# Taking a turn's outputs before the range steps of the next cosine argument

## The chip, the cores and the metric

One NeuronCore of a Trainium2 chip runs the whole program in one launch. The metric is device time in microseconds. The time before is 681.76 us, the median of 3 runs (681.07, 681.76 and 683.96).

## The reference, cut to what matters

Three stages follow each other on 1152 tokens (2 batches of 576) of width 512:

```
scores = q @ k.T / 8, kept for 0 <= i - j < 64      # sliding window attention, 8 heads of 64
x = softmax(scores) @ v                              # (1152, 512)

p = domain_probs / (sum(domain_probs) + 1e-9)        # 4 experts
x = sum over e of  p[:, e] * (relu(x @ w1[e]) @ w2[e])    # w1 512x1024, w2 1024x512

h = x @ w_in                                         # 512 -> 2048
out = (h * cos(h)) @ w_out                           # 2048 -> 512
```

## The kernel before, in words

Every product is done in three passes of a split format: each operand is a high part (fp32r) and a low part (the rest), and hi*hi + hi*lo + lo*hi are summed in PSUM. ScalarE makes the high parts by a copy (`w_hi` L418, `hp_hi` L423), VectorE or GpSimd the low parts by a subtraction (`hp_lo` L550 on VectorE, `w_lo` L314 on GpSimd).

After the attention the work goes in 18 turns of 3 token tiles (384 tokens each) by 6 blocks of weights: blocks 0 to 3 are the experts, blocks 4 and 5 are the two halves of the last layer (the cosine blocks). A turn is called (block, tile). It has 8 chunks of 128 hidden rows, and each chunk has an "up" product of 12 matmuls of 384 columns (L721) into one of four PSUM banks, and a "down" product (12 matmuls L749 in an expert turn, 9 matmuls of 512 columns L752 in a cosine turn) that adds to the turn's outputs in the other four banks. TensorE runs three chunks ahead: in its iteration f (0 to 7) of a turn it does the up product of chunk f+3, which for f of 5 and more belongs to the next turn, and then the down product of chunk f. I call the chunk whose up product is done in iteration f "the chunk of iteration f"; its down product comes three iterations later.

Within a cosine chunk the work passes between engines. ScalarE scales and rounds the argument (`c_u`, L428). VectorE does the three range steps: it takes the rounding constant off (`c_k`, L583), and subtracts the multiple of two pi in two parts (`c_r1` L585, `c_r2` L588). ScalarE takes the absolute value (L435) and the sine (L437), VectorE multiplies by h (`h_raw`, L596). The split of this chunk into `hp_hi` (ScalarE, L423) and `hp_lo` (VectorE, L550) is issued one iteration late: ScalarE does it behind the `c_u` of the following chunk, VectorE behind the following chunk's `c_r2`. All these orders are written out by hand, and each engine's queue is in order.

At the end of a turn VectorE moves the outputs from PSUM to the accumulator `acc` (`take_outputs`): a copy (L575) in the first block of a layer, an addition (L577) in the others, 4 pieces of 384 columns in an expert turn and 3 of 512 in a cosine turn. They wait for the turn's last down product (`down_done`). The first down product of the next turn waits for `y_taken` of the bank it writes, and for `hp_lo` of its chunk. In a turn followed by cosine work in its iteration 7 (these are (3,2), (4,0), (4,1), (4,2), (5,0) and (5,1)) `take_outputs` is called from inside `times_cosine`, between the previous chunk's `hidden_low` and the wait for the sine.

In the last tile of a block the next block's weights are refilled: ScalarE does `high_weights(f - 1)` in iteration f behind `hidden_high`, and ahead of the absolute value and sine; the eighth one, `high_weights(FC - 1)` (L456), comes behind the sine of iteration 7 and ahead of the next turn's first `c_u`. GpSimd makes each `w_lo` when its `w_hi` is there. Behind the eight `w_lo` of block 4, GpSimd also makes the input of the last layer for tile 2: `next_input(2)`, a cast to `x_hi` (L363) and a subtraction to `x_lo` (L365), both over 1536 columns. In front of block 4's eight it has done the same for tiles 0 and 1.

All tiles of the cosine steps (`c_u` to `c_cos`) and `acc` are parts of one SBUF tensor, so the profile calls them `arena`.

Of the kernel before, what the change touches and what calls it, by code (L numbers as in the profile page):

```python
# [34 lines left out]
FC = F1 // P  # L35
# [45 lines left out]
def build(nc, q, k, v, probs, weights, out):  # L81
    with ExitStack() as ctx:
# [418 lines left out]
        def _(dve):  # L501
# [46 lines left out]
            def hidden_low(f, s):  # L548
                dve.wait_ge(hp_hi_done, s + 1 + C_HI)
                nc.vector.tensor_tensor(hp_lo[:, f % HP, :], h_raw[:, f % HP, :], hp_hi[:, f % HP, :],  # L550
                                        ALU.subtract).then_inc(hp_lo_done, 1)
# [12 lines left out]
            def take_outputs(e, turn, t, mix, last=False):  # L564
                if isinstance(e, int) and e == E:
                    dve.wait_ge(x2_lo_done, t + 1)
                if not last:
                    dve.wait_ge(down_done, turn * FC + FC + C_DOWN)
                for c in range(DC if mix else OC):
                    if last:  # L570
                        dve.wait_ge(result_done, c + 1)
                    n = TOK if mix else DM
                    cell = acc[:, ds1(t), c * n:(c + 1) * n]
                    if isinstance(e, int) and e in (0, E):
                        nc.vector.tensor_copy(cell, y_ps[c][:, 0:n].unsqueeze(1)).then_inc(y_taken, 1)  # L575
                    else:
                        nc.vector.tensor_tensor(cell, y_ps[c][:, 0:n].unsqueeze(1), cell, ALU.add).then_inc(y_taken, 1)  # L577

            def times_cosine(f, s, late, take=None):
                n = s - MIX * FC  # L580
                bank_h = h_ps[f % HB][:, 0:TOK]
                dve.wait_ge(cos_u, n + 1)
                nc.vector.tensor_scalar_sub(c_k, c_u, ROUND).then_inc(cos_k, 1)  # L583
                dve.wait_ge(cos_k, n + 1)
                nc.vector.scalar_tensor_tensor(out=c_r1, in0=c_k, scalar=-TWO_PI_HI, in1=bank_h,  # L585
                                               op0=ALU.mult, op1=ALU.add).then_inc(cos_r1, 1)
                dve.wait_ge(cos_r1, n + 1)
                nc.vector.scalar_tensor_tensor(out=c_r2, in0=c_k, scalar=-TWO_PI_LO, in1=c_r1,  # L588
                                               op0=ALU.mult, op1=ALU.add).then_inc(cos_r, 1)
                if late:  # L590
                    hidden_low((f - 1) % FC, s - 1)
                if take is not None:
                    take_outputs(*take)
                dve.wait_ge(cos_done, n + 1)
                dve.wait_ge(hp_hi_done, s - HP + 1 + C_HI)
                nc.vector.tensor_tensor(h_raw[:, f % HP, :], c_cos, bank_h, ALU.mult).then_inc(h_taken, 1)  # L596

            def dve_turn(e, t, turn, mix_now, mix_next, last=False):
                for f in range(FC):
                    g, s = (f + LAG) % FC, turn * FC + f + LAG  # L600
                    own = f < FC - LAG
                    if last and not own:
                        if f == FC - LAG:
                            hidden_low(FC - 1, s - 1)
                    elif mix_now if own else mix_next:
                        wrap = isinstance(t, int) and t == NTOK - 1
                        share(g, s, e if own or not wrap else e + 1, t if own else 0 if wrap else t + 1)
                    else:
                        times_cosine(g, s, not (isinstance(s, int) and s == MIX * FC),
                                     (e, turn, t, mix_now) if f == FC - 1 else None)  # L610
                if mix_next or last:
                    take_outputs(e, turn, t, mix_now, last)
# [16 lines left out]
            for f in range(FC):  # L629
# [17 lines left out]
                if f != FIRST:  # L647
                    s = f + FIRST if f < FIRST else f + LAG
# [194 lines left out]
def ds1(i):  # L843
    return bass.ds(i, 1)
# [37 lines left out]
```

## Time and profile before

| what | value |
|---|---|
| median of 3 runs | 681.76 us (681.07 to 683.96) |
| the profiled execution's own time | 683.99 us |
| its span | 682.2 us |
| TensorE matmul busy | 649.3 us (95%), 3960 instructions |
| VectorE busy | 319.0 us (47%), 718 instructions |
| ScalarE busy | 237.7 us (35%), 511 instructions |
| GpSimd busy | 156.2 us (23%), 100 instructions |
| mean granted TensorE clock | 0.982 of full speed |
| chain that ended last, by engine | PE 90%, DVE 3%, ACT 3%, POOL 3%, issue 2% |

PE is TensorE, PEld its weight loads, DVE VectorE, ACT ScalarE, POOL GpSimd. Times in rows are in us from the start of the span unless marked ns. The span is 1.8 us shorter than the execution's own time. The cosine turns begin near 480 us; the last one ends with the span.

### The profile page before, as it was taken

What the parts mean: (1) busy time and instruction counts of PE and PEld (TensorE: products, weight loads), DVE (VectorE), ACT (ScalarE), POOL (GpSimd) and SP (SyncE); (2) the same over time, 40 slices, a digit from 0 to 9 for tenths busy, and PEclk for the clock granted to TensorE, in tenths of its full rate; (3) what the DMA queues carried; (4) which work ended last, traced back from release to release, by engine and by line L of the source; (5) the groups of instructions that cost most, each with busy time, mean ns of one, the idle gap of its engine ahead of it and who ended that gap; (6) DMA issues with size and microseconds to landing.
All of it is one profiled execution on the core that took longest, in us unless ns stands there. A gap on an engine that the chain in (4) does not pass through costs nothing.

```text
span 682.2 us, 10822 instructions
## 1 busy us (share of the span) xinstructions
PE 649.3 (95%) x3960; PEld 617.4 (91%) x3960; DVE 319.0 (47%) x718; ACT 237.7 (35%) x511; POOL 156.2 (23%) x100
## 2 busy tenths in 40 slices
PE   5867789999999999999999999999999999899998
PEld 4757679999999999999999999999899999799996
DVE  4542264232423232423232423234866688866664
ACT  5752352113211113311123211126455466544453
POOL 6632210005500015400015303055600025300000
PEclk9987899999999999999999999999999999899999
DMA  9961130003400003300004200003200003001011
GB/s 286 302 222 49 62 135 1 1 1 104 144 0 1 0 0 124 123 0 0 0 10 138 99 1 0 0 32 123 93 2 0 1 32 92 1 1 47 0 46 47
DMA packets 21684, 39.59 MB, mean 58 GB/s; under 512 B 2064, under 2 KB 13328, under 8 KB 21648
## 3 DMA queue, kind: packets, MB, share of 16 engines
q1 hardware_dynamic: 21564, 39.08, 17.6%
q8 instruction: 23, 0.38, 0.2%
q14 instruction: 13, 0.11, 0.1%
q10 hardware_dynamic: 84, 0.02, 0.0%
HBM read 36.72 MB, written 2.38 MB: 57 GB/s over the span
## 4 chain that ended last, share of the span: by engine, by line
PE 90%; DVE 3%; ACT 3%; POOL 3%; issue 2%; POOLq 0%; ACTq 0%; DVEq 0%
PE bank L721 43%; PE bank L749 29%; PE bank L752 14%; POOL w_lo L314 2%; PE bank L713 2%; PE bank L700 1%; ACT w_hi L418 1%; ACT arena L394 1%; DVE hp_lo L550 0%; PE bank L685 0%; POOL mask L291 0%; DVE arena L583 0%; DVE arena L588 0%; DVE arena L525 0%; DVE arena L577 0%
## 5 line engine op out<-in xcount | busy, mean ns | idle before, releaser
L721 PE MATMUL bank<-x_hi,w_hi 128*128 128x384 f32 (+1 forms) x576 | 197.7, 343 | 11.6 <-POOL w_lo L314 11.3
L721 PE MATMUL bank<-x_hi,w_lo 128*128 128x384 f32 (+1 forms) x576 | 195.3, 339 | 0.0
L721 PE MATMUL bank<-x_lo,w_hi 128*128 128x384 f32 (+1 forms) x576 | 195.1, 339 | 0.0
L314 POOL TENSOR_TENSOR w_lo<-w_raw,w_hi 128x1024 fp32r<-128x1024 f32 (+1 forms) x52 | 117.4, 2261 | 331.0 <-ACT w_hi L418 325.3
L423 ACT ACTIVATE hp_hi<-h_raw 128x384 fp32r<-128x384 f32 x144 | 75.0, 523 | 304.3 <-DVE h_raw L556 282.8
L556 DVE SCALAR_TENSOR_TENSOR h_raw<-bank,p_bc 128x384 f32<-128x384 f32 x96 | 53.3, 557 | 179.7 <-PE bank L721 178.7
L749 PE MATMUL bank<-hp_hi,w_hi 128*128 128x384 f32 x384 | 130.8, 341 | 1.8 <-DVE hp_lo L550 1.8
L749 PE MATMUL bank<-hp_lo,w_hi 128*128 128x384 f32 x384 | 128.9, 336 | 0.0
L749 PE MATMUL bank<-hp_hi,w_lo 128*128 128x384 f32 x384 | 128.8, 335 | 0.0
L721 PEld LDWEIGHTS bank<-x_hi,w_hi 128*128 128x128 f32 x576 | 109.9, 191 | 15.8 <-POOL w_lo L314 12.3
L550 DVE TENSOR_TENSOR hp_lo<-h_raw,hp_hi 128x384 fp32r<-128x384 f32 x144 | 91.1, 635 | 69.6 <-ACT hp_hi L423 69.6
L721 PEld LDWEIGHTS bank<-x_lo,w_hi 128*128 128x128 f32 x576 | 110.0, 191 | 1.9
L721 PEld LDWEIGHTS bank<-x_hi,w_lo 128*128 128x128 f32 x576 | 109.8, 191 | 0.0
L749 PEld LDWEIGHTS bank<-hp_hi,w_hi 128*128 128x128 f32 x384 | 72.7, 189 | 2.6 <-DVE hp_lo L550 2.0
L749 PEld LDWEIGHTS bank<-hp_lo,w_hi 128*128 128x128 f32 x384 | 72.7, 189 | 0.0
L749 PEld LDWEIGHTS bank<-hp_hi,w_lo 128*128 128x128 f32 x384 | 72.5, 189 | 0.0
L752 PE MATMUL bank<-w_hi,hp_hi 128*128 128x512 f32 x144 | 56.9, 395 | 4.4 <-DVE arena L575 2.8
L752 PE MATMUL bank<-w_lo,hp_hi 128*128 128x512 f32 x144 | 57.4, 399 | 0.0
L752 PE MATMUL bank<-w_hi,hp_lo 128*128 128x512 f32 x144 | 57.4, 398 | 0.0
L418 ACT ACTIVATE w_hi<-w_raw 128x1024 fp32r<-128x1024 f32 x44 | 46.1, 1047 | 0.1
L435 ACT ACTIVATE arena<-arena 128x384 f32<-128x384 f32 x48 | 25.2, 525 | 55.6 <-DVE arena L588 55.6
L596 DVE TENSOR_TENSOR h_raw<-arena,bank 128x384 f32<-128x384 f32 x48 | 26.5, 552 | 33.7 <-ACT arena L437 33.7
(46 smaller groups left out, 468.4 us busy)
## 6 DMA issues: line engine op xcount, KB each, us to landing
w_raw<-in_weights SPq DMA_DIRECT2D x44, 512.0 KB, 3.5
arena<-in_q SPq DMA_DIRECT2D x12, 192.0 KB, 4.8
p_bc<-p_scratch SPq DMA_DIRECT2D x4, 576.0 KB, 6.7
result<-arena SPq DMA_DIRECT2D x9, 256.0 KB, 2.1
w_raw<-in_weights SPq DMA_DIRECT2D x8, 256.0 KB, 5.6
arena<-in_k SPq DMA_DIRECT2D x8, 224.0 KB, 4.6
arena<-in_v SPq DMA_DIRECT2D x4, 384.0 KB, 3.6
arena<-in_v SPq DMA_DIRECT2D x4, 320.0 KB, 6.6
```

Of the source, the lines that this page charges most:

```text
L314: return nc.gpsimd.tensor_tensor(w_lo[:, f, cols], w_raw[:, f % STAGE, cols], w_hi[:, f, cols], ALU.subtract)
L394: last = nc.scalar.activation(prob[:, g % PR, t, :], s_sb[:, g % 2, t, :], ACT.Exp, bias=neg_max[:, g % PR, t:t + 1], scale=-1.0, accum_ou ...
L418: nc.scalar.activation(w_hi[:, f, :], w_raw[:, f % STAGE, :], ACT.Copy).then_inc(w_hi_done, 1)
L423: nc.scalar.activation(hp_hi[:, f % HP, :], h_raw[:, f % HP, :], ACT.Copy).then_inc(hp_hi_done, 1)
L435: nc.scalar.activation(c_abs, c_r2, ACT.Abs).then_inc(cos_abs, 1)
L550: nc.vector.tensor_tensor(hp_lo[:, f % HP, :], h_raw[:, f % HP, :], hp_hi[:, f % HP, :], ALU.subtract).then_inc(hp_lo_done, 1)
L556: nc.vector.scalar_tensor_tensor(out=h_raw[:, f % HP, :].unsqueeze(1), in0=ps[:, 0:TOK].unsqueeze(1), scalar=0.0, in1=p_bc[:, ds1(e), toke ...
L596: nc.vector.tensor_tensor(h_raw[:, f % HP, :], c_cos, bank_h, ALU.mult).then_inc(h_taken, 1)
L713: last = nc.tensor.matmul(o_bank(m)[heads, block_of * WIN:(block_of + 1) * WIN], v_w[:, r, WINDOW_OF[t][block_of], heads], prob_t[:, h, bl ...
L721: last = nc.tensor.matmul(ps[:, 0:TOK], w[:, f, chunk(c)], x[:, c, token_cols(t)], start=c == 0 and i == 0, stop=c == DC - 1 and i == 2)
L749: product = nc.tensor.matmul(y_ps[c][:, 0:TOK], w[:, f, DM + c * P:DM + (c + 1) * P], h[:, f % HP, :], **flags)
L752: product = nc.tensor.matmul(y_ps[c][:, :], h[:, f % HP, chunk(c)], w[:, f, DM:2 * DM], **flags)
```

## The change

`times_cosine` is called with `take` in iteration 7 of the six turns named above. There, the low part of the previous chunk and then the outputs are now done ahead of the three range steps; before, they came behind them. Nothing is added or removed, and no other engine's order is written differently.

```diff
             def times_cosine(f, s, late, take=None):
                 n = s - MIX * FC
                 bank_h = h_ps[f % HB][:, 0:TOK]
+                if take is not None:
+                    hidden_low((f - 1) % FC, s - 1)
+                    take_outputs(*take)
                 dve.wait_ge(cos_u, n + 1)
                 nc.vector.tensor_scalar_sub(c_k, c_u, ROUND).then_inc(cos_k, 1)
...
                 nc.vector.scalar_tensor_tensor(out=c_r2, in0=c_k, scalar=-TWO_PI_LO, in1=c_r1,
                                                op0=ALU.mult, op1=ALU.add).then_inc(cos_r, 1)
-                if late:
+                if late and take is None:
                     hidden_low((f - 1) % FC, s - 1)
-                if take is not None:
-                    take_outputs(*take)
                 dve.wait_ge(cos_done, n + 1)
```

## Rows read from the trace of the kernel before

**Rows 1.** Waits of PE from 440 us on: total us, times, longest us.
```profile
PE bank L752 <- DVE arena L575: 2.8, 1, 2.8
PE bank L752 <- DVE arena L577: 1.6, 1, 1.6
```
**Rows 2.** Timeline of PE, end of turn (3,2): start us, us, instruction, idle before.
```profile
479.82 0.34 PE L721 MATMUL bank<-x_hi,w_lo 128*128 128x384 f32 x1
481.71 0.47 PE L752 MATMUL bank<-w_hi,hp_hi 128*128 128x512 f32 x1 [1.55 <-DVE arena L577]
...
490.16 0.39 PE L752 MATMUL bank<-w_hi,hp_hi 128*128 128x512 f32 x1
```
**Rows 3.** Timeline of DVE, end of turn (3,2) and the two chunks after.
```profile
477.87 0.56 DVE L588 SCALAR_TENSOR_TENSOR arena<-arena 128x384 f32<-128x384 f32 x1
478.35 2.75 DVE L550 TENSOR_TENSOR hp_lo<-h_raw,hp_hi 128x384 fp32r<-128x384 f32 x1
481.02 1.94 DVE L577 TENSOR_TENSOR arena<-bank,arena 128x384 f32<-128x384 f32 x4
...
485.60 3.19 DVE L588 SCALAR_TENSOR_TENSOR arena<-arena 128x384 f32<-128x384 f32 x1
488.71 0.55 DVE L550 TENSOR_TENSOR hp_lo<-h_raw,hp_hi 128x384 fp32r<-128x384 f32 x1
```
**Rows 4.** Timeline of ACT, end of turn (3,2).
```profile
476.42 0.52 ACT L423 ACTIVATE hp_hi<-h_raw 128x384 fp32r<-128x384 f32 x1
...
479.02 0.62 ACT L437 ACTIVATE arena<-arena,half_pi 128x384 f32<-128x384 f32 x1
479.55 1.04 ACT L418 ACTIVATE w_hi<-w_raw 128x1024 fp32r<-128x1024 f32 x1
480.49 0.47 ACT L428 ACTIVATE arena<-bank 128x384 f32<-128x384 f32 x1
```
**Rows 5.** Timeline of POOL, end of turn (3,2).
```profile
477.96 5.39 POOL L314 TENSOR_TENSOR w_lo<-w_raw,w_hi 128x1024 fp32r<-128x1024 f32 x2 [0.93 <-ACT w_hi L418]
483.30 1.47 POOL L363 CAST x_hi<-arena 128x1536 fp32r<-128x1536 f32 x1
484.85 3.52 POOL L365 TENSOR_TENSOR x_lo<-arena,x_hi 128x1536 fp32r<-128x1536 f32 x1
```
**Rows 6.** Timeline of DVE, end of turn (4,1).
```profile
547.24 1.88 DVE L575 COPY arena<-bank 128x512 f32 x3
549.03 0.54 DVE L596 TENSOR_TENSOR h_raw<-arena,bank 128x384 f32<-128x384 f32 x1
```
**Rows 7.** Timeline of POOL in the refill of turn (4,2), two of its eight.
```profile
555.09 2.39 POOL L314 TENSOR_TENSOR w_lo<-w_raw,w_hi 128x1024 fp32r<-128x1024 f32 x1 [66.72 <-ACT w_hi L418]
...
571.93 2.39 POOL L314 TENSOR_TENSOR w_lo<-w_raw,w_hi 128x1024 fp32r<-128x1024 f32 x1 [0.65 <-ACT w_hi L418]
```
**Rows 8.** Timeline of DVE in the refill of turn (4,2) and at its end.
```profile
569.79 0.56 DVE L596 TENSOR_TENSOR h_raw<-arena,bank 128x384 f32<-128x384 f32 x1 [0.78 <-ACT arena L437]
...
572.13 2.60 DVE L588 SCALAR_TENSOR_TENSOR arena<-arena 128x384 f32<-128x384 f32 x1
...
575.98 0.55 DVE L596 TENSOR_TENSOR h_raw<-arena,bank 128x384 f32<-128x384 f32 x1 [0.77 <-ACT arena L437]
...
579.23 0.55 DVE L596 TENSOR_TENSOR h_raw<-arena,bank 128x384 f32<-128x384 f32 x1 [0.78 <-ACT arena L437]
...
584.54 1.87 DVE L575 COPY arena<-bank 128x512 f32<-128x512 f32 x3
```
**Rows 9.** Timeline of PE, end of turn (4,2).
```profile
582.09 0.34 PE L721 MATMUL bank<-x_hi,w_lo 128*128 x1
585.27 0.80 PE L752 MATMUL bank<-w_hi,hp_hi 128*128 128x512 f32 x1 [2.84 <-DVE arena L575]
...
588.98 0.34 PE L721 MATMUL bank<-x_hi,w_hi 128*128 x1
```
**Rows 10.** Windows: stretch, length, busy us of each engine, granted clock, DMA.
```profile
585.20:588.40 3.20, 3.13 (x7) 2.49 (x8) 3.20 (x5) 1.99 (x4) 2.03 (x1) 0.50 0.02 5
```

## The prediction

> **What bounds the kernel now.** I read the busy shares first (matmuls 95% of the span, the chain of waits 90% on PE), then PE's own waits behind 440 us, since only the six boundaries named in the change are touched, and then the timelines of PE, DVE, ACT and POOL at each of them. A DVE edit moves the time only where PE waits for DVE. Behind 440 us PE does so twice [rows 1]: 1.6 us at the end of turn (3,2), and 2.8 us at the end of turn (4,2). The reader should see in both that the first down product of the next turn waits for its bank to be taken. At the other four boundaries PE does not wait.
>
> Why DVE is late there is seen beside POOL. An `hp_lo` costs 0.55 us, but the one at 478.35 took 2.75: a POOL `w_lo` had begun at 477.96 [rows 3, 5]. A `c_r2` costs 0.56, but took 3.19 at 485.60, ending 0.42 behind the end (488.37) of the `x_lo` begun at 484.85 [rows 3, 5]. So a DVE step with both inputs in SBUF waits for the running POOL operation and ends 0.42 after it; `c_k` (one input, 0.36 long) is held too and, as in the profile's other cases, I take it to end 0.22 after. The `c_r2` at 477.87 had started when `w_lo` came, and the `hp_lo` asked for at 478.35, while that `c_r2` ran, was still served behind `w_lo`: an operation of POOL that arrives during a DVE step goes ahead of the DVE step behind it. The takes, which read PSUM, are not held: four in 1.94 us while `w_lo` ran.
>
> **Boundary (3,2) to (4,0), what is gained.** The last up product before the wait starts its last matmul at 479.82, and the next product would follow 0.17 behind, at 479.99; it came at 481.71 [rows 2]. With the change `hp_lo` needs only `hp_hi`, which is ready at 476.94 [rows 4], and ends near 477.5, ahead of `w_lo`. The takes start when the last down product is finished, about 478.2. The first takes about 0.55, so the bank is free by 478.8, ahead of 479.99. The whole 1.72 us goes: two up-down pairs took 490.16 - 481.71 = 8.45 [rows 2], so the third down product of the turn, that of the chunk of iteration 7, could start at 479.99 + 8.4 = 488.4.
>
> **The same boundary, what is late next.** The takes end at 480.1, and only then do the range steps come. `c_k` is asked for at 480.1 while `w_lo` runs from 477.96 to 480.35, and ends at 480.57. `c_r1` and `c_r2` (0.59 each from start to start) end at 481.75; absolute value and sine at 482.95. Behind this sine stands the last `w_hi` of the block: sine at 479.02 and `w_hi` at 479.55 before [rows 4], sine at 482.33 and `w_hi` at 482.86 after, so 3.3 us late. That is the price, for three things queue behind it. POOL's last `w_lo`, then its cast and `x_lo`, run one after another from there: `w_lo` 483.98 to 486.37, cast to 487.95, `x_lo` to about 491.75 (2.39, 1.5 and 3.7 with the gaps, of [rows 5] with a little for DVE steps between them). ACT's next `c_u` comes 0.94 behind `w_hi` [rows 4], at 483.8, and is ready at 484.27, too late to get `c_k` in before `w_lo`. So `c_k` ends at 486.59, `c_r1` at 487.18; `c_r2` is asked for during the cast and ends at 488.37; `x_lo` arrives during it, at 488.03, and goes ahead of the `hp_lo` behind it. This `hp_lo`, of the chunk of iteration 7, ends at 491.75 + 0.42 = 492.2. Before, it ended at 489.26 [rows 3], ahead of its use at 490.16. Now PE wants it at 488.4 and waits 3.8 us. That product starts at 492.2 instead of 490.16: +2.05 us, the 1.72 gained being already in it.
>
> The wait also touches the clock. In front of 585.27 PE had stood for 2.84 us, and behind it the granted clock was 0.50, that is 1.2 GHz, for 3.2 us [rows 9, 10]: nine matmuls took 588.98 - 585.27 = 3.71 instead of 2.08, so 1.63 us lost. In front of 481.71 it had stood for 1.55 and lost nothing of that kind (two pairs in 8.45). A wait of 3.8 is nearer to the first: I add 1.6; the ends are 0 and 3.3 (twice it).
>
> A rule of the Trainium skill bears on the held steps: SBUF — State Buffer, section Who interferes with whom, says that VectorE and GpSimd share a pair of ports, that whoever issues first has it for its whole instruction, and that the other blocks fully. The order in [rows 3, 5] agrees. By the rule taken at its word a held `hp_lo` would add its full 0.55 behind POOL and not 0.42; the sum of this boundary would then be about 0.4 higher for its three held steps.
>
> **The four boundaries without POOL work,** (4,0), (4,1), (5,0), (5,1): the takes start 0.25 earlier, which nobody waits for, and `h_raw` of that chunk comes 2.5 us later. At (4,1): takes at 547.0, `c_k` 1.79 later (547.24 to 549.03 [rows 6]) at 548.8, `h_raw` at 551.55 instead of 549.03. Its down product is three iterations of 4.19 later, with over 3 us to spare, and a late chain gains 0.9 us a chunk. Cost 0; were that cover gone, 2.5 each.
>
> **Boundary (4,2) to (5,0).** Here PE stands from 582.26 (0.17 behind 582.09) to 585.27, and with the clock this costs 4.6 us [rows 9]. Taken alone, the edit removes it: `hp_lo` and the first take would be done by 581.9. But the refill in turn (4,2) starts from a chain 2.5 us late, and I followed it chunk by chunk. A late chunk is of two kinds. Clear: `h_raw` to next `h_raw` 3.25 (575.98 to 579.23). Blocked: 6.19 (569.79 to 575.98), because `w_lo` begins 2.14 behind the first `h_raw` (571.93) and `c_r2` is asked for at 2.34 (572.13) [rows 7, 8]. The kinds alternate: the `w_lo` begun in a clear chunk holds the next one's `c_k` for a microsecond, which puts its `c_r2` behind the next `w_lo`. Before, the first `w_lo` came at 555.09 [rows 7] and iterations 3 and 5 were blocked; iteration 6 was clear, with `h_raw` at 579.23. After: iteration 7 of (4,1) 551.55, iteration 0 554.8, iteration 1 clear (the first `w_lo` starts only at 556.95) 558.05, 2 blocked 564.25, 3 clear 567.5, 4 blocked 573.7, 5 clear 576.9, 6 blocked 583.1. All these are still ahead of the down products that need them (the nearest by under 1 us). Then `hp_lo` at +1.14 and the take 0.47 behind: 584.7, where it was 584.54 [rows 8], and PE starts 0.73 later as before, at 585.4. So the gain is eaten by the refill, +0.1. The last `w_hi` is again 4 to 5 us late, but with nothing but one `w_lo` behind it: `hp_lo` of iteration 7 ends at 595.5 against a use at 595.25, +0.2. Bounds for the boundary: -4.6 (all of it) and +2.5 (one more blocked chunk's lateness reaching PE); I take +0.3.
>
> **Sum.** 2.05 + 1.6 + 0.3 = +3.9 us. Against the profiled execution's own 683.99 that is 687.9. The median of the runs shown is 2.2 below that execution; the difference is carried over: 681.76 + 3.9 = 685.7 us, +0.57%. About 0.5%, 3.4 us, is what a measurement can tell from no change.
>
> **Rivals.**
> 1. No clock loss behind the new wait: the same waits, +2.3, 684.1. For it: runs before differ by 2.9 us, so the clock may fall in some executions only. Against: the wait is longer than the one in [rows 9]. Chance 0.2.
> 2. Turn (4,2) ends in a clear chunk (one race of 0.2 us decides the alternation: `hp_lo` of the chunk of iteration 0 at 556.74 against `w_lo` at 556.95). Then PE's wait at 582.26 goes, and only about 1.0 us comes back at the third down product for a late `hp_lo`: -3.6 in place of +0.3. With the loss of the first boundary +0.1, 681.9. Chance 0.1.
> 3. Not slower: `hp_lo` gets the port ahead of `x_lo` near 488.4. It is asked for 0.26 behind `x_lo`; from about 488.0 on it would win. Then the third down product starts at 488.85 instead of 490.16, -1.3, no clock loss, and with +0.3 the time is 680.8. For it: `hp_lo` did get in between POOL operations at 480.6. Against: there it had been waiting first. Chance 0.12; together with rival 2 (-1.3 - 3.6) 676.9, chance 0.03.
> 4. The takes are moved and nothing changes at either place, because chains regain it: 681.8. Against: [rows 1] show PE waiting for exactly these takes. Chance 0.05.
>
> Forecast 0.5. Its own range is 684.2 to 687.8 (clock 0 to 3.3). The range for 8 in 10 is 680.2 to 687.8, leaving out the double gain. Slower by over 0.5%: 0.42 (most of the forecast's 0.5, the part with a full clock loss); within 0.5%: 0.5 (rivals 1, 2, 4, most of 3, the rest of the forecast); faster: 0.08.
>
> **What would show it.** Right: the take at the end of (3,2) starts near 478.2 and PE has no wait near 480; the sine-to-`w_hi` pair 3.3 us later; one PE wait of 3 to 4 us some 8 us after the boundary, for `hp_lo`, with clock 0.50 behind it; at the end of (4,2) the wait of nearly 3 us still there, about 4 us later in the span. Wrong: no wait at the third down product of (4,0); no wait at the end of (4,2); a wait at one of the four quiet boundaries.

## The result, and the profile after

The changed kernel takes 689.23 us (median of 6 runs, 686.31 to 690.17) against 682.77 us before (6 runs, 681.07 to 683.96): ratio 1.0093, 95% interval 1.0069 to 1.0117, so 6.4 us slower (4.7 to 8.0). A second comparison, with other executions, gave 688.24 against 683.42 us, ratio 1.0061 (1.0039 to 1.0084), 4.2 us. The kernel is slower; the forecast was 685.7 with a range to 687.8, so the sign was right and the time was missed.

| | before | after |
|---|---|---|
| profiled execution's own time, us | 683.99 | 689.13 |
| its span, us | 682.2 | 687.3 |
| mean granted clock | 0.982 | 0.978 |

Line numbers behind 582 move by 1 to 3: L721 is L722 now, L752 is L753, `c_k` L586, `c_r2` L591. Times near 480 us run 0.14 us ahead of those before.

PE's waits behind 440 us, to be held against [rows 1] (total us, times, longest us):

```profile
PE bank L753 <- DVE hp_lo L550: 3.6, 1, 3.6
PE bank L753 <- DVE arena L575: 3.1, 1, 3.1
```

The 1.6 us wait for the takes of (3,2) is gone and a wait of 3.6 us for an `hp_lo` has come; the one at the end of (4,2) is still there and slightly longer. PE's timeline behind the end of (3,2) answers to [rows 2]:

```profile
479.68 0.33 PE L722 MATMUL bank<-x_hi,w_lo 128*128 128x384 f32 x1
479.86 0.39 PE L753 MATMUL bank<-w_hi,hp_hi 128*128 128x512 f32 x1
...
488.06 0.34 PE L722 MATMUL bank<-x_hi,w_lo 128*128 128x384 f32 x1
491.99 0.50 PE L753 MATMUL bank<-w_hi,hp_hi 128*128 128x512 f32 x1 [3.60 <-DVE hp_lo L550]
...
495.28 0.52 PE L722 MATMUL bank<-x_hi,w_hi 128*128 128x384 f32 x1
```

The first down product of (4,0) follows at once, at 479.86. The third starts at 491.99, which is 1.97 us later than in [rows 2] on the clock of before (490.16 - 0.14 = 490.02). The reason reads off the other three engines, against [rows 3 to 5]. DVE:

```profile
476.83 0.56 DVE L550 TENSOR_TENSOR hp_lo<-h_raw,hp_hi 128x384 fp32r<-128x384 f32 x1 [0.87 <-ACT hp_hi L423]
477.98 1.95 DVE L577 TENSOR_TENSOR arena<-bank,arena 128x384 f32<-128x384 f32 x4 [0.58 <-PE bank L750]
479.84 0.61 DVE L586 TENSOR_SCALAR arena<-arena 128x384 f32<-128x384 f32 x1
...
484.20 2.28 DVE L586 TENSOR_SCALAR arena<-arena 128x384 f32<-128x384 f32 x1 [0.77 <-ACT arena L428]
486.52 0.56 DVE L588 SCALAR_TENSOR_TENSOR arena<-arena,bank 128x384 f32<-128x384 f32 x1
487.11 1.12 DVE L591 SCALAR_TENSOR_TENSOR arena<-arena 128x384 f32<-128x384 f32 x1
488.16 3.78 DVE L550 TENSOR_TENSOR hp_lo<-h_raw,hp_hi 128x384 fp32r<-128x384 f32 x1
```

ACT, the sine of iteration 7 and the eighth `w_hi` behind it:

```profile
482.23 0.62 ACT L437 ACTIVATE arena<-arena,half_pi 128x384 f32<-128x384 f32 x1
482.75 1.04 ACT L418 ACTIVATE w_hi<-w_raw 128x1024 fp32r<-128x1024 f32 x1
483.70 0.47 ACT L428 ACTIVATE arena<-bank 128x384 f32<-128x384 f32 x1
```

POOL:

```profile
477.83 2.41 POOL L314 TENSOR_TENSOR w_lo<-w_raw,w_hi 128x1024 fp32r<-128x1024 f32 x1 [0.92 <-ACT w_hi L418]
483.87 2.40 POOL L314 TENSOR_TENSOR w_lo<-w_raw,w_hi 128x1024 fp32r<-128x1024 f32 x1 [3.64 <-ACT w_hi L418]
486.22 1.60 POOL L363 CAST x_hi<-arena 128x1536 fp32r<-128x1536 f32 x1
487.90 3.62 POOL L365 TENSOR_TENSOR x_lo<-arena,x_hi 128x1536 fp32r<-128x1536 f32 x1
```

POOL now stands idle 3.64 us for a `w_hi` that ACT has behind the sine; `c_k`, `c_r2` and `hp_lo` are then held by one POOL operation each (2.28, 1.12 and 3.78 us for work of 0.36, 0.56 and 0.55).

At the end of (4,2), against [rows 8]: `h_raw` of iteration 6, the held `c_r2` ahead of it, and the take:

```profile
582.82 2.62 DVE L591 SCALAR_TENSOR_TENSOR arena<-arena 128x384 f32<-128x384 f32 x1
585.37 0.55 DVE L550 TENSOR_TENSOR hp_lo<-h_raw,hp_hi 128x384 fp32r<-128x384 f32 x1
586.68 0.55 DVE L597 TENSOR_TENSOR h_raw<-arena,bank 128x384 f32<-128x384 f32 x1 [0.77 <-ACT arena L437]
587.82 0.56 DVE L550 TENSOR_TENSOR hp_lo<-h_raw,hp_hi 128x384 fp32r<-128x384 f32 x1 [0.59 <-ACT hp_hi L423]
588.30 1.88 DVE L575 COPY arena<-bank 128x512 f32<-128x512 f32 x3
```

PE there, against [rows 9]:

```profile
585.57 0.34 PE L722 MATMUL bank<-x_hi,w_lo 128*128 x1
589.04 0.79 PE L753 MATMUL bank<-w_hi,hp_hi 128*128 128x512 f32 x1 [3.13 <-DVE arena L575]
...
593.04 0.52 PE L722 MATMUL bank<-x_hi,w_hi 128*128 x1
...
596.16 0.39 PE L753 MATMUL bank<-w_hi,hp_hi 128*128 128x512 f32 x1
```

And two windows behind both waits, against [rows 10] (length, busy us of PE, PEld, DVE, ACT and POOL, then the granted clock, DMA share, GB/s; 0.50 is half of full speed):

```profile
492.90:496.30 3.40, 3.40 (x11) 2.81 (x10) 2.48 (x6) 2.10 (x5) 0.00 (x0) 0.50 0.00 0
...
588.40:595.30 6.90, 6.26 (x17) 5.39 (x18) 4.82 (x8) 2.99 (x6) 2.86 (x2) 0.51 0.01 2
```

Half clock, 1.2 GHz, for 3.4 us behind the new wait and for nearly 6.9 us at the old one, the first 0.6 us of which PE still waits. Before, it had been 3.4 us there: [rows 10] show 3.2 of them, and this window of the kernel before the rest, up to 588.6:

```profile
588.00:589.00 1.00, 1.00 (x5) 0.82 (x4) 0.97 (x1) 0.00 (x0) 0.75 (x1) 0.69 0.00 0
```

**The 5.1 us between the two profiled executions** come apart like this. New wait: +1.97. Half clock behind it: nine plus twelve matmuls took 3.29 + 2.54 us for 2.08 + 2.10, +1.65. Wait at the end of (4,2): from 585.74 (0.17 behind 585.57) to 589.04 is 3.30 against 3.01, +0.29. Half clock behind it: 589.04 to 596.16 is 7.12 against 591.07 - 585.27 = 5.80, +1.32. Together 5.23, less 0.14 for the earlier start: 5.09, and the spans differ by 5.1.

### The profile page after: what moved, and what is told of

It is laid out like the page before. It is cut to its first block, busy times and chain, and to the rows that moved or that the text cites. A ratio compares the mean times of both kernels' runs of the same rounds, so it can differ in the third digit from the quotient of the medians.

```text
span 687.3 us, 10822 instructions
## 1 busy us (share of the span) xinstructions
PE 652.0 (95%) x3960; PEld 619.7 (90%) x3960; DVE 319.6 (47%) x718; ACT 237.1 (34%) x511; POOL 155.7 (23%) x100
## 4 chain that ended last, share of the span: by engine, by line
PE 86%; DVE 6%; ACT 3%; POOL 2%; issue 1%; DMA 1%; SPq 0%; ACTq 0%; DVEq 0%
PE bank L722 41%; PE bank L750 30%; PE bank L753 12%; POOL w_lo L314 2%; PE bank L714 2%; PE bank L701 1%; DVE arena L591 1%; ACT w_hi L418 1%; DVE arena L586 1%; ACT arena L437 1%; DVE hp_lo L550 1%; DMA arena<-in_k 1%; ACT arena L435 1%; PE bank L686 1%; DVE arena L577 1%
## 5 line engine op out<-in xcount | busy, mean ns | idle before, releaser
L722 PE MATMUL bank<-x_hi,w_hi 128*128 128x384 f32 (+1 forms) x576 | 198.4, 344 | 11.7 <-POOL w_lo L314 11.3
L722 PE MATMUL bank<-x_hi,w_lo 128*128 128x384 f32 (+1 forms) x576 | 195.8, 340 | 0.0
L722 PE MATMUL bank<-x_lo,w_hi 128*128 128x384 f32 (+1 forms) x576 | 195.6, 340 | 0.0
L722 PEld LDWEIGHTS bank<-x_hi,w_hi 128*128 128x128 f32 x576 | 110.6, 192 | 15.9 <-POOL w_lo L314 12.3
L550 DVE TENSOR_TENSOR hp_lo<-h_raw,hp_hi 128x384 fp32r<-128x384 f32 x144 | 87.8, 611 | 76.0 <-ACT hp_hi L423 76.0
L722 PEld LDWEIGHTS bank<-x_lo,w_hi 128*128 128x128 f32 x576 | 110.6, 192 | 2.0
L722 PEld LDWEIGHTS bank<-x_hi,w_lo 128*128 128x128 f32 x576 | 110.2, 191 | 0.0
L753 PE MATMUL bank<-w_hi,hp_hi 128*128 128x512 f32 x144 | 57.4, 398 | 6.7 <-DVE hp_lo L550 3.6
L753 PE MATMUL bank<-w_lo,hp_hi 128*128 128x512 f32 x144 | 58.1, 403 | 0.0
L753 PE MATMUL bank<-w_hi,hp_lo 128*128 128x512 f32 x144 | 58.0, 403 | 0.0
```

The costliest lines, as they stand in the source:

```text
L722: last = nc.tensor.matmul(ps[:, 0:TOK], w[:, f, chunk(c)], x[:, c, token_cols(t)], start=c == 0 and i == 0, stop=c == DC - 1 and i == 2)
L753: product = nc.tensor.matmul(y_ps[c][:, :], h[:, f % HP, chunk(c)], w[:, f, DM:2 * DM], **flags)
```

## Experiments

Each was timed beside the kernel before. A change in us is the ratio's distance from 1, times the median of the kernel before beside it (682.6 to 683.4 us); the 95% intervals reach 1 to 2 us to either side.

**only32, only42, block4: the change one place at a time.** `times_cosine` gets a flag `early`, true in iteration 7 of the chosen turns only:

```diff
-                if take is not None:
+                if take is not None and early:
                     hidden_low((f - 1) % FC, s - 1)
                     take_outputs(*take)
...
-                if late and take is None:
+                if late and not early:
                     hidden_low((f - 1) % FC, s - 1)
+                if take is not None and not early:
+                    take_outputs(*take)
```

> Early takes at the end of turn (3,2) alone; the other five boundaries as before. Theory (late sine delays the eighth w_hi, GpSimd's chain slides 3.3 us, the hp_lo of iteration 7 ends behind x_lo): no PE wait near 480, one of 3.6 us near 488.3 for hp_lo, 1.65 us of half clock behind it, so +3.6 us at this boundary; the wait at the end of (4,2) is that of the kernel before (3.0 us, for L575), with half clock behind it for 1.6 to 3 us: in all +3.6 to +5. Rival (all the loss is made at the end of (4,2)): +/-0.5 us or a gain of 1.7.

> Early takes at the end of turn (4,2) alone. Theory (there the change gains, and only a chain made late at (4,1) ate it): h_raw of iteration 6 near 579.2 as before, hp_lo and first take done by 581.9, no PE wait at 582.3, about 1 us of wait at the third down product of (5,0), no half clock: -3.6 us, -3 to -4.6. Rival (the wait there cannot be moved by the order of the takes): 0 +/- 0.5 us with the wait of 2.8 us in place.

> Early takes at the ends of (4,0), (4,1) and (4,2). Theory: the chain enters the refill of (4,2) 2.5 us late, h_raw of iteration 6 comes near 583 and is of the blocked kind, the wait at the end of (4,2) is 3.0 to 3.3 us: +0.1 to +0.5 us, up to +2 with a longer half clock. Rival (lateness at (4,1) is of no account): as the kernel with (4,2) alone, -3.6 us.

Measured: (3,2) alone 686.64 us, ratio 1.0052 (1.0037 to 1.0067), +3.5 us. (4,2) alone 679.45 us, ratio 0.9952 (0.9933 to 0.9971), -3.3 us. Block 4's three 683.46 us, ratio 1.0009 (0.9993 to 1.0026), +0.6 us. PE's waits behind 440 us, first of (4,2) alone:

```profile
PE bank L756 <- DVE arena L577: 1.6, 1, 1.6
PE bank L756 <- DVE hp_lo L550: 0.9, 1, 0.9
```

and of block 4's three:

```profile
PE bank L756 <- DVE arena L575: 3.1, 1, 3.1
PE bank L756 <- DVE arena L577: 1.6, 1, 1.6
```

With (4,2) alone the wait for L575 is gone and 0.9 us for `hp_lo` is left, which was the term of 1.0. With (4,0) and (4,1) early too, the wait is back at 3.1. So the same edit gains 3.3 us at one place, loses 3.5 at another, and the gain is lost when the takes of (4,0) and (4,1) are early too. All three rivals fall. That it is (4,1), 33 us ahead, whose lateness reaches the refill follows from the chunk-by-chunk reckoning; no run separates it from (4,0).

**whi_32: is it the sine in front of the eighth `w_hi`?** (3,2) alone, and in ScalarE's iteration 7 of that turn the eighth high part is issued ahead:

```diff
                 if refill is not None:
                     high_weights(*refill)
+                if eighth is not None:
+                    high_weights(*eighth)
                 act.wait_ge(cos_r, n + 1)
```

> Early takes at the end of (3,2) alone, and there the eighth w_hi goes ahead of the absolute value and the sine of iteration 7. Theory: POOL's w_lo, cast and x_lo run from about 480.4 without a gap and end near 488; hp_lo of iteration 7 ends near 489.9, PE waits for it 1.5 us at most and without half clock: -0.3 us against before, 3.6 us or more under the kernel with (3,2) alone. Rival (the loss is from the takes themselves standing ahead of the range steps, not from the eighth w_hi): the same +3.6 us as with (3,2) alone.

Measured: 682.51 us, ratio 0.9996 (0.9978 to 1.0014), -0.3 us. The loss of 3.5 us is gone with the takes still early. PE's wait there:

```profile
PE bank L759 <- DVE hp_lo L553: 1.6, 1, 1.6
```

It is 1.6 us long and no half clock follows. So the loss of 3.5 us comes from what ACT has queued behind the sine. The 1.6 us that are left use up what the early takes gained: x_lo, begun at 483.13, still meets the chain, now at the `c_k` of iteration 7, which takes 3.44 us from 483.43.

**split_after: is it x_lo that holds `hp_lo`?** The changed kernel with

```diff
-                nc.gpsimd.tensor_tensor(x_lo[cell], whole, x_hi[cell], ALU.subtract).then_inc(x2_lo_done, 1)
+                for c in range(DC):
+                    piece = nc.gpsimd.tensor_tensor(x_lo[:, c, token_cols(t)], whole[:, c, :],
+                                                    x_hi[:, c, token_cols(t)], ALU.subtract)
+                piece.then_inc(x2_lo_done, 1)
```

> The changed kernel with GpSimd's x_lo (one subtraction over 1536 columns) done in four of 384. Theory (hp_lo of iteration 7 waits for the whole of x_lo, since x_lo is asked for first): it gets in behind the first piece, near 489.5, PE's wait at the third down product of (4,0) is 1.0 to 1.8 us instead of 3.6 and no half clock follows: 3.5 to 4 us under the changed kernel, +2.5 us against before. Rival (hp_lo is late by its own chain, or by the cast): the wait stays 3.6 us, +6.4 us.

Measured: 682.54 us, ratio 1.0002 (0.9987 to 1.0017), +0.1 us. Its DVE, POOL and PE in turn:

```profile
487.44 1.12 DVE L594 SCALAR_TENSOR_TENSOR arena<-arena 128x384 f32<-128x384 f32 x1
488.49 1.35 DVE L553 TENSOR_TENSOR hp_lo<-h_raw,hp_hi 128x384 fp32r<-128x384 f32 x1
```
```profile
488.23 4.87 POOL L366 TENSOR_TENSOR x_lo<-arena,x_hi 128x384 fp32r<-128x384 f32 x4
```
```profile
489.90 0.50 PE L756 MATMUL bank<-w_hi,hp_hi 128*128 128x512 f32 x1 [1.16 <-DVE hp_lo L553]
```

`hp_lo` gets in behind the first piece and ends at 489.84; the wait is 1.2 us instead of 3.6. The mechanism is the one expected, but the gain is 2.4 us larger than I wrote: I had reckoned from the changed kernel's 6.4, in which the longer half clock at the end of (4,2) is contained. Here that place shows 3.4 us of it, as before, though its wait is 3.1 us; that is 1.3 of the 2.4. The rest is not explained; against the 4.2 of the second comparison the gain is 4.1, near the 3.5 to 4 expected.

**fill_after and fill_before: what is the clock's share?** TensorE gets 12 spare matmuls ahead of a wait, written to a bank that the next up product starts afresh: in fill_after ahead of the third down product of (4,0) and of the first of (5,0), in fill_before ahead of the latter only. TensorE's loop over (5,0) and (5,1) is written out for it:

```diff
+                    if f == fill:
+                        pe.wait_ge(h_taken, s + 1 - HB + 1 + C_H)
+                        up_cells(h_ps[(g + 1) % HB], g, t, range(DC))
                     down(f, turn * FC + f, turn, mix, last)
...
-                    with pe.Fori(0, NTOK - 1) as t:
-                        pe_turn(e, t, e * NTOK + t, False)
+                    for t in range(NTOK - 1):
+                        pe_turn(e, t, e * NTOK + t, False, fill=0 if t == 0 else None)
```

> The changed kernel, with TensorE given 12 spare matmuls of 384 columns ahead of the two waits (third down product of (4,0), first of (5,0)); what they write is overwritten. TensorE's two turns (5,0) and (5,1) are unrolled for it. Theory (of the +6.4 us, 2.3 are longer waits and the rest is half clock behind them): no half clock behind either place, the same starts of the products, 2.1 us of each wait filled: 1.65 and 2.95 us come back, 4 to 5 us under the changed kernel, +1.5 to +2.5 us against before. Rival (the clock is of no account, the chain of VectorE is all): as the changed kernel, +6.4 us.

> The kernel before, with TensorE given 12 spare matmuls of 384 columns ahead of the first down product of (5,0), whose result is overwritten; turns (5,0) and (5,1) unrolled on TensorE. Theory (half clock follows the 2.8 us wait there in most executions and costs 1.6 us): no half clock near 585, -1.6 us against before, or -1 us where hp_lo of the third down product is late then. Rival (the clock falls there seldom outside the profiled execution): 0 +/- 0.5 us.

Measured: fill_after 686.85 us, ratio 1.0058 (1.0034 to 1.0082), +4.0 us; fill_before 681.73 us, ratio 0.9965 (0.9946 to 0.9985), -2.4 us. In fill_after PE at the end of (4,2) reads:

```profile
586.36 0.47 PE L753 MATMUL bank<-w_hi,hp_hi 128*128 128x512 f32 x1 [1.17 <-DVE arena L575]
...
596.39 0.50 PE L753 MATMUL bank<-w_hi,hp_hi 128*128 128x512 f32 x1 [1.44 <-DVE hp_lo L550]
```

The nine matmuls from 586.36 take 2.14 us, so the clock does not fall, but PE at full speed then meets the third down product 1.44 us ahead of its `hp_lo`. In the profiled executions fill_after runs 95.59 us from the third down product of (4,0) to the first of (5,0), and the changed kernel 97.05; from there to the end 97.06 and 98.23. So in the profiled executions spare matmuls give back 2.6 us, not the 4.6 that I expected: at the end of (4,2) the half clock had been covering a late `hp_lo`. The timed runs do not confirm even that: +4.0 lies between the two expectations, 2.4 below the changed kernel's first timing and only 0.2 below its second. fill_before is clearer. Its profile runs 95.36 us from the first product of (5,0) to the end, against 96.90 in the kernel before; the nine matmuls there take 2.14 for 3.71 us, which is the whole difference, so writing out the loop costs nothing visible. Timed, it gains 1.0 to 3.7 us, more than the rival's 0.5. The half clock there is not rare: all eight profiled executions with a wait of 2.8 to 3.1 us at that place (of before, changed twice, only32, block4, whi_32, split_after and all_but32) show it.

**all_but32: are block 5's boundaries free?** The flag `early` is false in (3,2) only.

> Early takes everywhere but at the end of (3,2). Theory (the boundaries in block 5 are free): as the kernel with block 4's three alone, +0.6 us against before, no further PE wait. Rival (they cost some of the 6.4 that the parts measured so far, 3.6 and 0.6, do not add up to): +1.5 to +3 us.

Measured: 683.12 us, ratio 1.0002 (0.9988 to 1.0017), +0.1 us, with the same two waits (3.1 and 1.6) as block 4's three. Within the noise of about 1 us they are free.

**after_again: the changed kernel's time against its clock.**

> The changed kernel once more, for its time against the granted clock of every execution. Theory (2.3 us are longer waits, the rest is half clock): executions with the same mean clock as ones of the kernel before are 2 to 3 us slower, and the mean clock lies lower, 0.978 against 0.982 to 0.985; in all +5 to +7 us. Rival (something else than clock and the two waits): over 4 us slower at equal clock.

Measured: 688.24 us, +4.2 us as told above. By mean granted clock, executions of the kernel before and of the changed one (both comparisons):

```
clock    before, us (count)      changed, us (count)
0.987    681.0 (2)               -
0.985    682.3 (17)              -
0.982    683.9 (10)              -
0.983    -                       686.3, 686.7 (2)
0.980    -                       687.1 to 688.2 (4)
0.979    684.5 (2)               -
0.978    -                       688.7 to 690.2 (9)
0.977    686.0 (3)               -
```

The before column has the means of the runs beside only32. A step of 0.002 to 0.003 in the mean clock goes with 0.6 to 1.6 us. The changed kernel's executions lie at 0.978 to 0.983, most of those before at 0.982 and 0.985. At a clock between 0.977 and 0.979 the changed kernel is 3.9 us above this column (689.26 against 685.40), but its runs in after_again are only 2.8 above those of before beside them (688.94 against 686.16): my 2 to 3 is neither confirmed nor excluded.

The mean clock does not say where a stretch lies, and here the second profile of the changed kernel (687.14 us, mean clock 0.980) helps. It has the same two waits with half clock behind each, and runs the same 195.3 us from the third down product of (4,0) to the end. But that product starts at 490.09 instead of 491.99. Most of the 1.9 us are lost early: from 41 to 50 us, 60 matmuls took 5.7 us at a granted clock of 0.75 in the first profile, and 4.2 us at 0.91 in the second. The profile of the kernel before has the slow kind of that stretch too (0.76). Nothing in the change touches it. So the two profiled executions compare like with like there, and their 5.1 us are what the change does when both have it; the timed 6.4 and 4.2 us also hold how often each kernel happened to have the slow stretch, which the mean clocks cannot tell apart.

**combo and best: can both gains be had?** Early takes at (3,2) and (4,2) only, the eighth `w_hi` ahead in both; best has x_lo in four pieces as well.

> Early takes at the ends of (3,2) and (4,2) alone, and in both the eighth w_hi ahead of the absolute value and sine of iteration 7. Theory: -0.3 us from (3,2), -3.3 from (4,2) as measured alone, and the 0.9 us wait of (5,0)'s third down product gone as well: -4 to -5 us against before. Rival (the two places trade with each other through the lateness of the chain): no better than (4,2) alone, -3.3 us.

> Early takes at the ends of (3,2) and (4,2) alone, the eighth w_hi ahead of absolute value and sine there, and x_lo in four pieces. Theory (what is left there is the 1.6 us wait for hp_lo behind x_lo): c_k, c_r2 and hp_lo each get in between two pieces, the wait falls to 0.5 us or less: 1 to 1.6 us under the kernel without the pieces, -6 to -6.5 us against before. Rival (POOL's extra 1.3 us for four pieces and the three held steps give it back): no better than without the pieces, -4.9 us.

Measured: combo 677.77 us, ratio 0.9928 (0.9907 to 0.9949), -4.9 us; best 676.28 us, ratio 0.9889 (0.9859 to 0.9920), -7.6 us. In combo PE's only wait behind 440 us is this; in best none is left there.

```profile
PE bank L759 <- DVE hp_lo L553: 1.6, 1, 1.6
```

Both beat the kernel before and the changed one.

## Why the prediction was wrong, step by step

- **What is gained at (3,2): right.** The product came at 479.86 where 479.99 less the 0.14 shift was written.
- **What is late next: right in each link.** Sine 482.23, `w_hi` 482.75, `w_lo` 483.87, `c_k` end 486.48, `c_r2` end 488.23, `hp_lo` end 491.94, each within 0.15 us of the hand reckoning on that clock; +1.97 for +2.05. whi_32 and split_after show the two links (the `w_hi` behind the sine, x_lo ahead of `hp_lo`) by taking each away.
- **The clock behind the new wait: right,** +1.65 for +1.6.
- **The held steps:** `hp_lo` ended 0.42 behind x_lo (491.52), so the whole 0.55 that the Trainium skill's SBUF — State Buffer, Who interferes with whom, would have put there is not seen, while its order (who comes first holds the other out) is: x_lo, begun at 487.90, kept out the `hp_lo` that came at 488.16.
- **The four boundaries without POOL work: right** in that none has a wait of its own. all_but32 against block4's three shows it for block 5; for (4,0) and (4,1) it holds at the place itself, and the chain made late there is the next point.
- **The end of (4,2): the chain was right, the clock term was not.** The kinds alternate as written, iteration 6 is blocked, and the take started at 588.30, that is 584.82 once the 3.48 us of shift are taken off, for 584.7. But I held the half clock behind that wait at its size of before, and took +0.2 for a late `hp_lo` in its place. The trace shows 6.9 us of half clock for 3.4, and with it a boundary of +1.6 us (0.29 of wait, 1.32 of clock) where the sum had +0.3. This is the term of the sum that was mis-sized. The late `hp_lo` was reckoned rightly: it ended at 599.07, that is 595.59 for 595.5, but under the longer half clock its product came only at 600.34. only42 and block4 confirm that early takes ahead of (4,2) are what eats the gain.
- **Carrying the difference of 2.2 us over to the median was wrong too.** The profiled execution before has the slow stretch near 41 to 50 us, and a mean clock of 0.982 where half of the runs of before have 0.985 and 1.6 us less; the changed kernel's profiled execution has that stretch as well and is at its own median (689.13 and 689.23). 683.99 + 3.9 + 1.3 gives 689.2. Of the 2.2 us, 1.0 is that the median of three runs, 681.76, was low: with six it is 682.77. In the second comparison, where before has 683.42, the change costs 4.2 us, near the 3.9 written; that nearness is partly luck, since the mis-sized term is in that kernel's profile as well.

Rival 1 (no clock loss) and rivals 2 to 4 did not occur. The range failed at its upper end, since it let the clock fall further at the new wait only. That end is also not the sum of its terms, which give 684.1 to 687.4 and not 684.2 to 687.8. Every sign named as right came true, because none of them asked how long the half clock at the end of (4,2) would last.

**Open.** Why the half clock at the wait of (4,2) lasted 6.9 us in both profiled executions of the changed kernel but 3.4 us in those of block4, all_but32, split_after and only32, with waits of 3.1 us in the first three and 2.8 in the last. The parts only32 and all_but32 add up to 3.6 us; the whole measured 6.4 and 4.2, and the intervals do not say whether the rest is this longer half clock or the slow stretch near 41 to 50 us.

## What to carry to other kernels

When a step is moved behind another, read what stands behind it in the queue of the engine that waits for it: here three range steps held back a sine, the sine a weight copy, the copy GpSimd's chain, and that chain held up the one VectorE result that TensorE wanted 10 us later. An edit that is applied by rule at all places of a kind should be tried place by place: one gained 3.3 us, one lost 3.5, the other four were neutral or spoilt the gain of another. A wait of about 3 us on TensorE should be priced with the half clock behind it, in the kernel before as well, and the profiled execution's clock compared with that of the other runs before its time is carried over to a median.

## What the runs showed of the hardware that was not expected

The half clock at a wait has no fixed length: 3.4 us with 2.84 us of wait (before), 6.9 us with 3.13 us (changed), and again 3.4 us with the same 3.13 us in block4. No half clock followed the waits of 1.2 to 1.6 us. The price of a half clock can also be hidden: with the clock kept up by spare matmuls, 1.44 us of the time saved went into a wait that the slow matmuls had covered. And VectorE's `hp_lo` got in between the pieces of x_lo: four pieces of 384 columns instead of one of 1536 cut its time from 3.78 to 1.35 us, for 4.87 instead of 3.62 us on GpSimd.
